# First products of an MLP split by token column and set between the attention units of the opening

## The reference, cut to what matters

```python
def _attn_ref(q, k, v):                      # q, k, v: 4 x 8 x 576 x 64, float32
    B, H, S, D = q.shape
    window = 64
    scores = np.matmul(q, k.transpose(0, 1, 3, 2)) / np.sqrt(D)
    rel = pos[:, None] - pos[None, :]
    mask = (rel >= 0) & (rel < window)
    scores = np.where(mask, scores, -1e9)
    ...                                      # softmax over the last axis
    return np.matmul(attn, v)

x = attn_out as tokens x (heads * dim)       # 2304 x 512
x = (sigmoid(x @ moe_w_gate) * (x @ moe_w_val)) @ moe_w_out     # 512 -> 1536 -> 512
return ((x @ moe2_w_a) * (x @ moe2_w_b)) @ moe2_w_out           # 512 -> 1536 -> 512
```

## Time and profile before

| | us |
|---|---|
| median of 3 runs (947.07 to 947.95) | 947.08 |
| the profiled execution | 949.11 |
| its span | 947.3 |
| PE busy | 932.6 (98%) |
| DVE busy | 624.6 (66%) |
| ACT busy | 473.3 (50%) |
| POOL busy | 183.1 (19%) |

### The profile page before, as it was taken

One profiled execution on the slowest core, in us unless ns is written; L12 is line 12 of the kernel. 1 busy time (PEld: TensorE's weight loads), 2 busy tenths in 40 slices (PEclk: granted clock), 3 DMA queues, 4 the chain that ended last, 5 costly groups with the idle time before them and its releaser, 6 DMA issues.

```text
span 947.3 us, 17015 instructions
## 1 busy us (share of the span) xinstructions
PE 932.6 (98%) x6294; PEld 863.1 (91%) x6294; DVE 624.6 (66%) x1296; ACT 473.3 (50%) x944; POOL 183.1 (19%) x267
## 2 busy tenths in 40 slices
PE   6999999999999999999999999999999999999998
PEld 4899988888888888888899999999999999999998
DVE  6678686566755667646657557758575758664757
ACT  6778685467665767524334334334344525334232
POOL 4153333243234233333433000000000000000000
PEclk9999999999999999999999999999999999999999
DMA  9859969768948846946783287666796766867663
GB/s 226 213 186 283 263 200 304 203 199 224 274 151 242 257 117 186 317 143 200 267 319 119 106 329 272 251 249 226 287 357 245 262 223 246 318 252 266 230 245 134
DMA packets 147042, 222.37 MB, mean 235 GB/s; under 512 B 80656, under 2 KB 101648, under 8 KB 144656
## 3 DMA queue, kind: packets, MB, share of 16 engines
q1 hardware_dynamic: 130016, 170.42, 54.6%
q0 software_dynamic: 15200, 50.34, 16.5%
q10 hardware_dynamic: 1744, 0.52, 0.2%
HBM read 178.78 MB, written 42.47 MB: 234 GB/s over the span
## 4 chain that ended last, share of the span: by engine, by line
PE 95%; DVE 0%; issue 0%; ACT 0%; DVEq 0%
PE ps L651 16%; PE ps L653 15%; PE ps L652 15%; PE ps L772 14%; PE ps L770 14%; PE ps L771 14%; PE ps L643 2%; PE ps L608 2%; PE ps L619 1%; PE ps L594 1%; PE ps L595 1%; DVE probs_a L1105 0%; ACT probs_a L843 0%; DVE acc L1341 0%; DVE row_inv L1101 0%
## 5 line engine op out<-in xcount | busy, mean ns | idle before, releaser
L651 PE MATMUL ps<-x_hi,gv_hi 128*128 128x512 f32 (+1 forms) x480 | 179.0, 373 | 0.0
L653 PE MATMUL ps<-x_hi,gv_lo 128*128 128x512 f32 (+1 forms) x480 | 176.8, 368 | 0.0
L652 PE MATMUL ps<-x_lo,gv_hi 128*128 128x512 f32 (+1 forms) x480 | 176.7, 368 | 0.0
L770 PE MATMUL ps<-xc,wc 128*128 128x384 f32 x504 | 170.2, 338 | 0.0
L771 PE MATMUL ps<-xc,wc 128*128 128x384 f32 x504 | 170.2, 338 | 0.0
L772 PE MATMUL ps<-xc,wc 128*128 128x384 f32 x504 | 170.2, 338 | 0.0
L1245 DVE TENSOR_TENSOR tt<-ps,tt 128x384 f32<-128x384 f32 x108 | 59.1, 555 | 83.5 <-PE ps L772 83.2
L232 POOL DMA_DIRECT2D w_raw<-in_moe_w_gate x60 | 45.5, 759 | 332.8 <-DVE wo_lo L1139 322.6
L772 PE MATMUL ps<-wc,hc_lo 128*128 128x256 f32 x378 | 106.9, 283 | 0.0
L770 PE MATMUL ps<-wc,hc_hi 128*128 128x256 f32 x378 | 106.9, 283 | 0.0
L771 PE MATMUL ps<-wc,hc_hi 128*128 128x256 f32 x378 | 106.9, 283 | 0.0
(11 more groups left out here) (102 smaller groups left out, 1676.9 us busy)
## 6 DMA issues: line engine op xcount, KB each, us to landing
wc<-wprep SPq DMA_DIRECT2D x54, 1024.0 KB, 6.9
wc<-wprep SPq DMA_DIRECT2D x54, 768.0 KB, 5.8
wprep<-p_out SPq DMA_DIRECT2D x18, 1792.0 KB, 7.6
w_raw<-in_moe_w_gate POOLq DMA_DIRECT2D x60, 256.0 KB, 3.6
w_raw<-in_moe_w_val POOLq DMA_DIRECT2D x60, 256.0 KB, 4.1
w_raw<-in_moe_w_out POOLq DMA_DIRECT2D x60, 256.0 KB, 4.3
v_nat<-in_v SPq DMA_DIRECT2D x58, 128.0 KB, 5.6
q_nat<-in_q SPq DMA_DIRECT2D x48, 96.0 KB, 4.5
```

Of the source, the lines that this page charges most:

```text
L651: pe.matmul(dst, w_h, m_h, start=first, stop=False)
L652: pe.matmul(dst, w_h, m_l, start=False, stop=False)
L653: return pe.matmul(dst, w_l, m_h, start=False, stop=last)
L770: pe.matmul(dst, s_h, m_h, start=opens, stop=False, skip_group_check=True)
```

## The change

Nine things, all in the opening:

- step 0's gate and value products are made by `up_first(col, pair, side)`: one token column (192 of the 384 tokens), one pair of k tiles, one side; six matmuls of 192 columns each, eight calls, 48 matmuls in place of 24 of 384 columns. They are set between the turns and mixes, each waiting for the x and the weight piece that it needs;
- they also wait for `maxed` of all four doubles, since their banks held scores;
- the fill of double 4 moves from chunk 0 to behind mix(1), into bank 2 and 3, and waits for its q and k;
- the fill of double 3 moves in front of turn(0,1);
- a second buffer `turned_b` for turned probabilities, so that ACT's copy waits for the mix before the last and not for the last;
- DVE counts each split piece (`first_lo`), and the four pieces stand between masks, normalises and `mix_lo`;
- DVE masks first[1] unit 0 ahead of its second normalise of first[0], and unfills first[3] earlier;
- ACT copies k of doubles 2 and 3 earlier, and makes both exponentials of double 3 before the turned copy (2,1);
- ACT's and DVE's work for double 4 (k copy, unfill) and the split of step 0's `wo` move from chunk 0 into the lists.

```diff
+        turned_b = place("turned_b", A_H_HI, [P, 2, UB * P])
...
-                self.fill_bank = n % 2 * 2 if early else ATT_BANK
+                self.fill_bank = n % 2 * 2 if early else 2 if n == FIRST_DOUBLES else ATT_BANK
...
+                self.turned = turned_b if early and n % 2 else probs_t
...
             def fill(d):
                 pe.wait_ge(qk_in[d.qk_buf], QK_IN * d.qk_loads)
-                if not d.early:
+                if d.n == FIRST_DOUBLES:
+                    pe.wait_ge(unfilled, d.n)
+                    pe.wait_ge(k_copied, d.n)
+                elif not d.early:
                     pe.wait_ge(turned_out, 2 * d.n)
...
+            def up_first(col, pair, side):
+                if side == 1 and pair == 1:
+                    pe.wait_ge(gv_lo_ready, 1)
+                else:
+                    pe.wait_ge(first_lo, 2 * side + pair + 1)
+                pe.wait_ge(mixed_lo, 2 * col + pair + 1)
+                pe.wait_ge(maxed, 2 * FIRST_DOUBLES)
+                at = RING_AT + col * UQ
+                for t in (2 * pair, 2 * pair + 1):
+                    cols = slice((side * KT + t) * P, (side * KT + t + 1) * P)
+                    mm = three_products(bank((GATE_BANK, VALUE_BANK)[side], col * UQ, (col + 1) * UQ),
+                                        gv_hi[:, 0, cols], gv_lo[:, 0, cols],
+                                        x_hi[:, t, at:at + UQ], x_lo[:, t, at:at + UQ],
+                                        col == 0 and t == 0, col == FIRST_COLS - 1 and t == KT - 1)
+                if col == FIRST_COLS - 1 and pair == 1:
+                    mm.then_inc((gated, valued)[side], 1)
...
             score(first[1])
             turn_unit(first[0], 0)
+            fill(first[3])
             turn_unit(first[0], 1)
             score(first[2])
-            fill(first[3])
...
             mix(first[1])
+            fill(Double(FIRST_DOUBLES))
             turn_unit(first[2], 1)
+            up_first(0, 0, 0)
             turn_unit(first[3], 0)
             mix(first[2])
             turn_unit(first[3], 1)
+            up_first(0, 0, 1)
+            up_first(0, 1, 0)
             mix(first[3])
-            pe.wait_ge(mixed_lo, 3)
-            pe.wait_ge(maxed, 2 * FIRST_DOUBLES)
-            for side in range(2):
-                up_tiles(0, 0, side, RING_AT, WIDTHS[0], range(2))
+            up_first(0, 1, 1)
+            up_first(1, 0, 0)
+            up_first(1, 0, 1)
+            up_first(1, 1, 0)
+            up_first(1, 1, 1)
...
             def turned_copy_unit(d, r):
                 act.wait_ge(turned, 2 * d.n + r + 1)
-                if d.n >= 1:
-                    act.wait_ge(mixed, d.n)
-                act.copy(probs_t[:, r, :], bank(ATT_BANK + r, 0, UB * P)).then_inc(turned_out, 1)
+                if d.n >= 2:
+                    act.wait_ge(mixed, d.n - 1)
+                act.copy(d.turned[:, r, :], bank(ATT_BANK + r, 0, UB * P)).then_inc(turned_out, 1)
...
             normalise(first[2], 1, 1)
+            split_first(0)
             mask_and_max(first[3], 1)
```

More of the change, by code:

```diff
@@ L186, in attention_mlp_program @@
         mixed, mixed_hi, mixed_lo = sem("mixed"), sem("mixed_hi"), sem("mixed_lo")
-        gv_hi_ready, gv_lo_ready = sem("gv_hi_ready"), sem("gv_lo_ready")
+        gv_hi_ready, gv_lo_ready, first_lo = sem("gv_hi_ready"), sem("gv_lo_ready"), sem("first_lo")
         wo_hi_ready, wo_lo_ready = sem("wo_hi_ready"), sem("wo_lo_ready")
@@ L601, in score @@
                 pe.wait_ge(k_copied, d.n + 1)
-                if d.early and d.n >= 1:
+                if not d.early:
+                    pe.wait_ge(turned_out, 2 * d.n)
+                elif d.n >= 1:
                     pe.wait_ge(maxed, 2 * d.n)
@@ L644, in mix @@
                                            d.v[:, i, head],
-                                           probs_t[:, r, i * P + p * QB:i * P + (p + 1) * QB],
+                                           d.turned[:, r, i * P + p * QB:i * P + (p + 1) * QB],
                                            start=True, stop=True)
@@ L653, in three_products, with up @@
                 return pe.matmul(dst, w_l, m_h, start=False, stop=last)
-            def up_tiles(s, f, side, x_off, w, tiles):
+            def up_first(col, pair, side):
[14 more added lines that the diff above has]
+                    mm.then_inc((gated, valued)[side], 1)
+            def up(s, f, side, x_off, w, mixes=None):
+                if mixes:
+                    pe.wait_ge(mixed_lo, mixes)
                 pe.wait_ge(gv_hi_ready, s + 1)
@@ L660, in up_tiles @@
                 dst = bank((GATE_BANK, VALUE_BANK)[side], 0, w)
-                for t in tiles:
+                for t in range(KT):
                     cols = slice((side * KT + t) * P, (side * KT + t + 1) * P)
@@ L699, in chunk @@
                             fill(d)
-                    up(s, f, 0, x_off, w, mixes)
+                    if s > 0:
+                        up(s, f, 0, x_off, w, mixes)
                     mixes = None
-                    if d:
-                        score(d) if f == 0 and s > 0 else fill(d)
-                    up(s, f, 1, x_off, w)
+                    if d and s > 0:
+                        score(d) if f == 0 else fill(d)
+                    if s > 0:
+                        up(s, f, 1, x_off, w)
                     if d and (f > 0 or s == 0):
@@ L929, in chunk @@
                         split_gv(c, f + 1)
-                    split_wo(s, f)
+                    if s > 0:
+                        split_wo(s, f)
                     open_gate(s, w)
-                    if d and (f > 0 or s == 0):
+                    if d and f > 0:
                         copy_k(d)
@@ L1047, in _ @@
             copy_k(first[1])
+            copy_k(first[2])
             exps(first[0], 1)
-            copy_k(first[2])
             turned_copy_unit(first[0], 0)
             exps(first[1], 0)
+            copy_k(first[3])
             turned_copy_unit(first[0], 1)
             exps(first[1], 1)
-            copy_k(first[3])
             exps(first[2], 0)
@@ L1059, in _ @@
             mix_hi(first[0])
+            turned_copy_unit(first[2], 0)
             exps(first[3], 0)
-            turned_copy_unit(first[2], 0)
+            exps(first[3], 1)
             turned_copy_unit(first[2], 1)
-            exps(first[3], 1)
             mix_hi(first[1])
+            turned_copy_unit(first[3], 0)
             mix_hi(first[2])
-            turned_copy_unit(first[3], 0)
             turned_copy_unit(first[3], 1)
+            act.wait_ge(gv_hi_ready, 1)
+            copy_k(Double(FIRST_DOUBLES))
+            split_wo(0, 0)
             mix_hi(first[3])
-            act.wait_ge(gv_hi_ready, 1)
             for c in range(CHUNKS):
@@ L1133, in split_first @@
                                       ALU.subtract)
-                if i == 3:
-                    d.then_inc(gv_lo_ready, 1)
+                d.then_inc(gv_lo_ready if i == 3 else first_lo, 1)
             def split_wo(s, f):
@@ L1386, in _ @@
             unfill(first[2])
+            mask_and_max(first[1], 0)
             normalise(first[0], 1, 1)
-            mask_and_max(first[1], 0)
             mask_and_max(first[1], 1)
             normalise(first[1], 0, 1)
+            unfill(first[3])
             mask_and_max(first[2], 0)
             mask_and_max(first[2], 1)
-            unfill(first[3])
             normalise(first[1], 1, 1)
@@ L1397, in _ @@
             normalise(first[2], 1, 1)
+            split_first(0)
             mask_and_max(first[3], 1)
+            mix_lo(first[0])
             normalise(first[3], 0, 1)
-            mix_lo(first[0])
+            split_first(1)
             normalise(first[3], 1, 1)
+            split_first(2)
             mix_lo(first[1])
             mix_lo(first[2])
-            for i in range(4):
-                split_first(i)
+            split_first(3)
+            unfill(Double(FIRST_DOUBLES))
+            split_wo(0, 0)
             mix_lo(first[3])
```

## The result

| | changed kernel | kernel before |
|---|---|---|
| median, runs taken side by side | 950.23 us (7 runs, 948.58 to 950.81) | 947.95 us (7 runs, 947.07 to 949.18) |
| ratio | 1.0027, 95% interval 1.0017 to 1.0036 | |
| profiled execution | 949.94 us | 949.11 us |
| start of score(4) in it | 35.93 us | 35.10 us |

The change makes the kernel slower by 0.27%, 2.3 us by the medians. I had forecast 947.3 and no measurable change. The time lies 0.03 us above my range (944.8 to 950.2), and the whole interval of the ratio lies on the slower side, which I had given 0.25. Four of the seven runs of the kernel before in this table took 947.95 us or more; beside the experiments its medians are 947.09 to 947.19, and against those the change costs about 3.1 us (0.33%).

A forecast was written before the change was run, and what follows sets the result against it. TensorE (PE), busy 98% of the span, was taken as the bound. Fill at 24.3 us plus 9.3 of work and 1.7 of low clock put score(4) at 35.3, 0.2 later: 947.3 us, range 944.8 to 950.2.

The forecast's parts named there:

- the slower side: Whole kernel: slower by over 0.2%, the outcome of rivals 2 and 3 together; chance 0.25.
- PE behind 41 us is a full queue: PE from 41 us on is busy 902.69 of 906.30 us, so the kernel's time moves by what score(4) moves by.
- The fill waits for k: Fill of double 4 behind mix(1): PE waits for the last k load, fill at 24.3 us; chance 0.50.
- The price of a 192-column product: Step 0's split products on PE: 0.110 us each (0.090 to 0.118), 48 taking 5.3 us against 4.2 before.
- the sum: PE from fill to score(4): 24.3 + 9.3 of work + 1.7 low clock = 35.3 us, against 35.10 before.
- Rival 2: Step 0's products: 192 columns cost 0.175 us each, 3.1 us more in all, 950.4 us; chance 0.15.
- How late k is: Double 4's last k load: landed at 24.03 us before; earlier step 1 weights delay it 0 to 0.9, taken as 0.3.
- One low stretch, 1.7 us: PE from 24.1 us on: the wait brings one stretch at half clock, costing 1.7 us.
- rival 3: PE behind the wait: clock low for a second stretch and k 0.6 us later still, 949.6 us; chance 0.10.
- The same shift on the median gives 947.3 us: Whole kernel: score(4)'s shift of 0.2 us later, added to the median of 947.08 us.

The follow-up runs named there:

- experiment 1: Changed kernel with one line moved: the fill of double 4 stands in front of mix(3), not behind mix(1); 946.6 us, ratio 0.9990 to the kernel before.
- experiment 2: Changed kernel with SP's q and k loads of double 4 issued ahead of the v loads of doubles 2 and 3; 946.0 us, ratio 0.9981 to the kernel before.
- experiment 4: Kernel before with only the fill of double 4 moved behind mix(1); 949.56 us, ratio 1.0022 to the kernel before.
- experiment 3: Kernel before with only SP's q and k loads of double 4 put ahead of the v loads of doubles 2 and 3; 947.21 us, ratio 1.0002.
- experiment 5: Kernel before with step 0's 24 products made as 48 of 192 columns in the same place; 948.44 us, ratio 1.0016 to the kernel before.
- experiment 7: Changed kernel with POOL's weights of step 1 issued about as late as in the kernel before; 948.93 us, ratio 1.0020 to the kernel before.
- experiment 6: Changed kernel with useless PE work before the fill of double 4: 16 matmuls 948.56 us (1.0014), or 16 transposes 948.03 us (1.0011), against the kernel before.
- experiment 10: Kernel before, unchanged, profiled a second time; 947.02 us.
- experiment 8: Changed kernel without split or early products, fill before mix(3): 946.38 us (0.9992); same with double 4's k loaded early: 947.23 us (0.9996), against the kernel before.

## Why the prediction was wrong, point by point

**PE behind 41 us is a full queue, and the time moves by what score(4) moves by: right, and better than I claimed.** In all fourteen profiled executions the time is the start of score(4) plus 914.0 to 914.4: 35.10 and 949.11, 35.93 and 949.94, 31.61 and 945.63, 37.05 and 951.06, 33.06 and 947.02.

**The fill waits for k, and the products' gap is spent waiting: right.** I had the fill at 24.3, it started at 24.29. Experiments 1, 2 and 4 show it from three sides, and 3 is the control.

**The price of a 192-column product, 0.110 in a range of 0.090 to 0.118: right,** 0.112; experiment 5 confirms the sum. Rival 2 is gone.

**How late k is: right, and so close by luck.** I took the issue from one execution; in the ten profiles of experiment 7 it lies between 16.4 and 18.4 us and the landing between 22.7 and 24.9. And the weights cost about 0.9 us, not 0.3; in the changed kernel's profile an early issue made up for it.

**One low stretch, 1.7 us: mis-sized.** The clock was at half from 22.9 to 29.75. From the fill to score(4) PE took 35.93 - 24.29 = 11.64 us against the 9.3 of my sum: 2.3 us in place of 1.7, which gives 35.93 for my 35.3. The work itself was a little cheaper than I had it: in the profile with matmuls of experiment 6, all at the high clock, it took 34.33 - 25.24 = 9.09 us. So the low clock cost about 2.5. This is rival 3 in part.

**"The same shift on the median gives 947.3 us": this is the step that failed.** My shift was the difference between two executions with a low clock, since the earlier trace rows has two low stretches. The median was of another kind. The sum compared the changed kernel with a base that had already lost 2 us to the clock, and the result was added to a median that had not. The profiled execution took 949.11 where the median was 947.08, and I wrote both numbers down without asking what the 2 us were. Experiment 10 shows what they are: the median execution has no low stretch and score(4) at 33.06. Against that the sum of the prediction itself, 35.3, is 2.2 us later, and 947.08 + 2.2 = 949.3; with the low clock at its true size, 35.93, it is 947.08 + 2.9 = 950.0, where 950.23 was measured. So the change did two things. It added some time of its own: kept at work during the wait (experiment 6), PE lost 0.8 and 1.4 us to the kernel before. And it made a low clock behind the wait the rule (seven of seven runs), where in the kernel before the clock fell in 12 of 88; left idle, PE lost 2.3 us beside the kernel before and 3.1 against its usual 947.1. The second part is the larger. Rival 2 had come out at 950.4, above the range that I gave, and its time is close to the measured one by chance: its cause, dear short products, is not there.

What stays open: what decides, in a single execution, whether the clock falls. Stretches with nearly the same busy time (1.75 and 1.76 of 3.42 us) were followed by a low clock once and by a high one once. Whether the share of such executions differs from chip to chip was not tested either: in the three sets of runs the clock fell in 7 of 30, 1 of 33 and 4 of 25 runs of the kernel before.

## What to carry to other kernels

Work drawn ahead on an in-order queue brings its loads' landing time with it: before moving a step forward, look up when its last operand lands, and move the load first (one moved line of SP's list turned +0.27% into -0.19%). A wait on TensorE costs more than its length if it lets the clock fall, and then everything that piled up behind it runs at half speed. Work set into a wait can pay through the clock even where it saves no time of its own (experiments 6 and 8). And when the profiled execution lies off the median, find the rows that make the difference before adding anything to the median.

## What the runs showed of the hardware that I had not expected

- The same program on the same inputs takes about 947.1 us in most executions and 0.5 to 2.3 us more in a quarter of them (24 of 88). Two profiles show the clock in the opening as the difference: 0.996 and 1.000 over the span, 2.09 us. A first rise of the clock at about 18.5 us (experiment 3), where the other thirteen profiles have it by 15, is the likely source of the runs near 948.2 with a mean clock of 1.00; the column of the granted clock says 1.00 there, and only the durations show it.
- With the DMA engines full (shares of 0.95 to 1.26 from 13.87 to 24.1 us), a 96 KB load landed 5.8 to 6.8 us after its issue in five profiles, and 6.5 to 8.1 us after it in the five where 768 KB of other loads went out 2 to 3 us sooner; it landed 0.9 us later in the mean.
- A 192-column float32r product costs 0.112 us at the high clock, nearly as much as one of 256 columns (0.118), but 0.215 at the low one, where 384 columns take 0.32: below 256 columns little is saved at the high clock; at the low one no row has 256 columns. The weight load, 0.11 at the high clock, is the likely floor; this was not tested apart.
- A plain float32 matmul of 128 columns is recorded as two, 0.24 us together, a transpose of the same size as one of 0.12.
